# Low parts of all weights on VectorE, a split first weight block, and own slot sequences at both ends of a fused convolution and two-layer kernel

## The chip, the cores and the metric

One core of one Trainium2 chip runs the whole program. The time is that of one execution on the device, in microseconds (us); less is better. Three runs of the kernel before gave 2374.93, 2377.0 and 2377.89 us, so a median of 2377.0 us.

## What is computed

The reference, cut to what matters (`x` is 4 x 4096 x 192, so 16384 tokens of 192 values; the hidden size F is 2048; all float32):

```python
w = softmax(weight)                 # 8 heads, 7 taps
x = causal 7-tap convolution of x along the sequence, one set of taps per group of 24 channels
h = x @ w_in;  x = (h * cos(h)) @ w_out          # layer one, 192 -> 2048 -> 192
h = max(x @ w2_in, 0);  out = (h * h) @ w2_out   # layer two, 192 -> 2048 -> 192
```

## The kernel before

The tokens are cut into 32 tiles of 512 (`TOK`). Channels stand on the partitions; since 192 = 128 + 64, each operand has a main part of 128 rows and a side part of 64.

**Split products.** Every float32 product is made of products of a high and a low part. The high part is a copy of the value in the matmul's type (ScalarE, `ACT.Copy`), the low part is the value minus its high part (a subtraction). Weights are split once: `up_hi`, `up_lo`, `up_side` for the up projection, `dn_hi`, `dn_lo`, `dn_side` for the down projection, with suffix A for layer one and B for layer two. The low parts are made by VectorE for most of layer one (`layer1_up_lo`, `layer1_down_lo`) and by GpSimd for the side of layer one's up weights and for all of layer two (`late_lo_part`). Activations are split for every tile: `g_hi` on ScalarE (L615), `g_lo` on VectorE (L717), and likewise the layer inputs `xin_hi`, `xin_lo`, `xin_side`, `xin_odd`.

**Slots.** The program runs in turns. Turn i works on layer one of tile i (A), layer two of tile i-1 (B), reads and transposes the rows of tile i+1 (X), and transposes back the result of tile i-2 (Y). Turn -1 is the preparation of tile 0, turns 32 and 33 finish layer two and the output. A turn is a list of 18 slots: A 0 to 7 and B 0 to 7, each for two of the 16 blocks of the hidden dimension, and one X and one Y. `SLOTS` gives the order, and `FIRST_SLOTS` that of turns -1 and 0. A slot that doesn't run is passed over. On every engine the instructions stand in program order, slot by slot; semaphores tie the engines together. Turns 3 to 30 are a hardware loop, the others are written out.

**What an engine does in a slot.** TensorE makes the up products of the slot's pair into one of two PSUM buffers `h` (18 matmuls, each of 64 rows by 512 columns) and, interleaved with them on the other half of the rows, the down products (20 matmuls) of the pair that stood four slots earlier (`LAG`). Where only one of the two is there, it runs alone (`up_alone`, `down_alone`) and the two halves of the array overlap in part; `two_up_and_down` joins two ups with one down, and waits for what the second up needs between its steps. ScalarE reads `h` (L594 for A; L596 and the square L598 for B), makes the cosine (L604) one slot later and the high part (L615) two slots later. VectorE makes the fraction of a turn (L703, L705), then the product with the cosine (L712) in the next slot and the low part (L717) in the one after. So three engines pass each A pair round: ScalarE L594, VectorE L703 and L705, ScalarE L604, VectorE L712, ScalarE L615, VectorE L717, TensorE.

**The convolution.** Seven taps on the main and seven on the side part (`tap`, L736 to L744) stand in the slots of `TAP_SLOTS` (`FIRST_TAP_SLOTS` in turns -1 and 0). At `SPLIT_SLOT`, 16, ScalarE copies `x_side_A`, `x_odd` and `x_hi_A` (L651 to L653) and `split_layer1` on VectorE makes `x_lo_A` and the low rows of `x_side_A` (L750, L752); that sets `x1_made`, on which the first up product of the next turn waits. In the same way `split_layer2`, at slot 0, turns layer one's result `y_A` into layer two's input (L759 to L768) and sets `x2_made`, on which B 0 waits.

**The ends.** In turn -1 `layer1_hi` and `late_hi(0)` make the high parts of layer one's weights on ScalarE, as one block each. Layer two's weights come through one staging buffer, `late`: half of the up weights, the other half, the down weights. `late_hi` (ScalarE, at `LATE_SLOTS` of turn 0) and `late_lo_part` (GpSimd) empty it, then SP's queue loads the next part (L293 to L300). In turn 32 only B and Y run, in the places that `SLOTS` gives them.

## Time and profile before

| | |
|---|---|
| median of 3 runs | 2377.0 us |
| profiled execution, its own time | 2377.48 us |
| its span, first to last instruction | 2375.7 us |
| TensorE busy | 2315.7 us (97%), 20352 matmuls |
| VectorE busy | 1902.8 us (80%), 2125 instructions |
| ScalarE busy | 1776.5 us (75%), 1872 instructions |
| GpSimd busy | 24.0 us (1%), 11 instructions |
| mean granted TensorE clock | 0.990 of 2.4 GHz |

The profiled execution is 0.5 us above the median. Busy time of TensorE counts a matmul that runs alone on half of the rows as much as two side by side, so busy is not the same as full. The first two of 40 slices (59.4 us each) show TensorE 0.5 and 0.7 busy, all later ones 0.9 or more but the last (0.8). DMA is 31% busy in the first slice, 10% in the second, and next to nothing after.

### The profile page before, as it was taken

To read this page: it belongs to the slowest core of one execution; us is meant where nothing else is said; L and a number is where in the kernel's file an instruction comes from. 1 tells how busy PE (TensorE), PEld (TensorE's weight loads), DVE (VectorE), ACT (ScalarE), POOL (GpSimd) and SP (SyncE) were. 2 spreads that over 40 slices of the span, in tenths; PEclk is the share of its full clock that TensorE was granted. 3 is DMA by queue.
4 is the path that set the end of the run, shared out by engine and by line. 5 is a ranking of instruction groups with operands and counts; after the bars stand their busy time and mean duration, and the time that the engine had idled before them with its cause. 6 is when DMAs were issued, how large, how long until landed. Compare 5 with 4: busy or idle time off the path is not lost.

```text
span 2375.7 us, 49089 instructions
## 1 busy us (share of the span) xinstructions
PE 2315.7 (97%) x20352; PEld 2163.2 (91%) x20352; DVE 1902.8 (80%) x2125; ACT 1776.5 (75%) x1872; POOL 24.0 (1%) x11
## 2 busy tenths in 40 slices
PE   5699999999999999999999999999999999999998
PEld 4489999999999999999999999999999999999886
DVE  7788788888778878778888878888878888878861
ACT  5377777777777777777777777777777777777764
POOL 1200000000000000000000000000000000000000
PEclk9799999999999999999999999999999999999999
DMA  3100000000000000000000000000000000000000
GB/s 109 37 8 8 14 14 7 13 13 7 13 13 7 13 13 7 13 13 7 13 13 7 13 13 7 13 13 7 13 13 13 7 13 7 13 13 7 7 8 14
DMA packets 39308, 33.05 MB, mean 14 GB/s; under 512 B 1516, under 2 KB 38508, under 8 KB 39020
## 3 DMA queue, kind: packets, MB, share of 16 engines
q1 hardware_dynamic: 39100, 32.58, 4.6%
q8 instruction: 25, 0.41, 0.1%
q14 instruction: 7, 0.06, 0.0%
q10 hardware_dynamic: 176, 0.00, 0.0%
HBM read 19.99 MB, written 12.58 MB: 14 GB/s over the span
## 4 chain that ended last, share of the span: by engine, by line
PE 95%; DVE 3%; ACT 1%; issue 0%; DMA 0%; SPq 0%; ACTq 0%; DVEq 0%
PE h L349 10%; PE h L353 9%; PE h L351 9%; PE h L355 9%; PE y_A L394 6%; PE y_B L388 5%; PE y_B L394 5%; PE y_A L396 5%; PE y_B L396 5%; PE y_B L392 5%; PE y_A L388 5%; PE y_B L390 5%; PE y_A L392 4%; PE y_A L390 4%; PE h L357 3%; PE h L359 2%
## 5 line engine op out<-in xcount | busy, mean ns | idle before, releaser
L717 DVE TENSOR_TENSOR g_lo<-g,g_hi 128x1024 fp32r<-128x1024 f32 x512 | 626.7, 1224 | 200.3 <-ACT g_hi L615 196.4
L615 ACT ACTIVATE g_hi<-g 128x1024 fp32r<-128x1024 f32 x512 | 538.2, 1051 | 49.8 <-DVE g L712 49.5
L604 ACT ACTIVATE w<-w,quarter 128x1024 f32<-128x1024 f32 x256 | 295.5, 1154 | 281.6 <-DVE w L705 281.6
L349 PE MATMUL h<-x_side_A,up_side_A 64*128 64x512 f32 x1024 | 401.6, 395 | 38.2 <-DVE x_side_A L752 29.4
L388 PE MATMUL y_A<-g_hi,dn_lo_A 64*128 64x512 f32 x1024 | 407.5, 398 | 5.1 <-DVE g_lo L717 4.9
L388 PE MATMUL y_B<-g_hi,dn_lo_B 64*128 64x512 f32 x1024 | 405.4, 396 | 2.9 <-DVE g_lo L717 2.4
L394 PE MATMUL y_A<-g_hi,dn_side_A 64*128 64x512 f32 x1024 | 404.8, 395 | 0.0
L349 PE MATMUL h<-x_side_B,up_side_B 64*128 64x512 f32 x1024 | 399.2, 394 | 3.7 <-issue 3.6
L390 PE MATMUL y_A<-g_hi,dn_hi_A 64*128 64x512 f32 x1024 | 402.5, 393 | 0.0
L396 PE MATMUL y_B<-g_lo,dn_side_B 64*128 64x512 f32 x1024 | 400.2, 391 | 0.0
L390 PE MATMUL y_B<-g_hi,dn_hi_B 64*128 64x512 f32 x1024 | 400.2, 391 | 0.0
L396 PE MATMUL y_A<-g_lo,dn_side_A 64*128 64x512 f32 x1024 | 398.9, 390 | 0.0
L394 PE MATMUL y_B<-g_hi,dn_side_B 64*128 64x512 f32 x1024 | 398.4, 389 | 0.2
L392 PE MATMUL y_A<-g_lo,dn_hi_A 64*128 64x512 f32 x1024 | 398.3, 389 | 0.0
L351 PE MATMUL h<-x_hi_A,up_lo_A 64*128 64x512 f32 x1024 | 397.5, 390 | 0.0
L353 PE MATMUL h<-x_lo_A,up_hi_A 64*128 64x512 f32 x1024 | 397.4, 390 | 0.0
L392 PE MATMUL y_B<-g_lo,dn_hi_B 64*128 64x512 f32 x1024 | 397.2, 388 | 0.0
L355 PE MATMUL h<-x_hi_A,up_hi_A 64*128 64x512 f32 x1024 | 397.0, 389 | 0.0
L353 PE MATMUL h<-x_lo_B,up_hi_B 64*128 64x512 f32 x1024 | 393.5, 388 | 0.0
L351 PE MATMUL h<-x_hi_B,up_lo_B 64*128 64x512 f32 x1024 | 393.4, 388 | 0.0
L355 PE MATMUL h<-x_hi_B,up_hi_B 64*128 64x512 f32 x1024 | 393.3, 388 | 0.0
L594 ACT ACTIVATE g<-h 128x1024 f32<-128x1024 f32 x256 | 261.0, 1019 | 128.8 <-PE h L355 127.9
(96 smaller groups left out, 6261.0 us busy)
## 6 DMA issues: line engine op xcount, KB each, us to landing
rows_in<-x SPq DMA_DIRECT2D x32, 384.0 KB, 3.2
...
taps<-weight ACTq DMA_DIRECT2D x4, 0.7 KB
```

Of the source, the lines that this page charges most:

```text
L349: mm = pe.matmul(dst, up_side[kind][rows, f], xin_side[kind][rows, :], start=rows is top, stop=z)
L351: mm = pe.matmul(dst, up_lo[kind][rows, f], xin_hi[kind][rows, :], start=False, stop=z)
L353: mm = pe.matmul(dst, up_hi[kind][rows, f], xin_lo[kind][rows, :], start=False, stop=z)
L355: mm = pe.matmul(dst, up_hi[kind][rows, f], xin_hi[kind][rows, :], start=False, stop=z)
L388: mm = pe.matmul(y[kind][:, 0, :], dn_lo[kind][rows, c, :], hi, start=a, stop=False)
L390: mm = pe.matmul(y[kind][:, 0, :], dn_hi[kind][rows, c, :], hi, start=False, stop=False)
L392: mm = pe.matmul(y[kind][:, 0, :], dn_hi[kind][rows, c, :], lo, start=False, stop=z)
L394: mm = pe.matmul(y[kind][:, 1, :], dn_side[kind][rows, c, :], hi, start=a, stop=False)
L396: mm = pe.matmul(y[kind][:, 1, :], dn_side[kind][rows, c, :], lo, start=False, stop=z)
L604: act.activation(v, v, ACT.Sin, bias=quarter[:, 0:1], scale=-TURN).then_inc(cosine, 1)
L615: act.activation(g_hi[:, r, :, :], g[:, r, :, :], ACT.Copy).then_inc(hi_made[kind], 1)
L717: dve.tensor_tensor(g_lo[:, r, :, :], g[:, r, :, :], g_hi[:, r, :, :].bitcast(F32), ALU.subtract).then_inc(lo_made[kind], 1)
```

## The change

Low parts: the GpSimd block is gone. `late_lo_part` and the subtraction for the side rows of layer one's up weights now stand on VectorE. `late_lo_part(1)`, `(2)` and `(3)` come at slots 8, 11 and 17 of turn 0 (`LATE_LOW_SLOTS`), and `late_hi` moves on ScalarE from slots 9, 12, 15 to 7, 10, 14.

Split block: layer one's up weights are prepared in two parts, the first 512 columns (pairs 0 and 1) and the other 1536. In turn -1 all main taps come before all side taps, ScalarE copies the first part, then `x_hi_A` after the main taps, then the sides, and only then the second part and `late_hi(0)`. TensorE waits for the first part at A 0 and for the second at A 2. The weights are staged in `w` and a new buffer `stage_in_side` instead of `g`.

Input split, in every turn: ScalarE now makes `x_hi_A` first and the two side copies after it, with two increments of `x1_hi`; VectorE makes `x_lo_A` after the first and `x_side_A` after the second.

Slot sequences: `FIRST_SLOTS` and `FIRST_TAP_SLOTS` are changed (turn 0 has its A pairs one slot earlier, X between A 2 and A 3, one tap per slot from 9 to 15), and `LAST_SLOTS` is new, for turns 32 and 33.

```diff
-FIRST_SLOTS = [("B", 0), ("B", 1), ("B", 2), ("B", 3), ("B", 4), ("Y", 0), ("A", 0), ("A", 1), ("A", 2),
-               ("A", 3), ("X", 0), ("A", 4), ("A", 5), ("A", 6), ("A", 7), ("B", 5), ("B", 6), ("B", 7)]
+FIRST_SLOTS = [("B", 0), ("B", 1), ("B", 2), ("B", 3), ("Y", 0), ("A", 0), ("A", 1), ("A", 2), ("X", 0),
+               ("A", 3), ("A", 4), ("A", 5), ("A", 6), ("A", 7), ("B", 4), ("B", 5), ("B", 6), ("B", 7)]
+
+LAST_SLOTS = [("A", 0), ("B", 0), ("B", 1), ("B", 2), ("B", 3), ("B", 4), ("B", 5), ("B", 6), ("B", 7),
+              ("Y", 0), ("A", 1), ("A", 2), ("A", 3), ("A", 4), ("A", 5), ("A", 6), ("A", 7), ("X", 0)]
...
-FIRST_TAP_SLOTS = (11, 11, 12, 13, 14, 15, 15)
+FIRST_TAP_SLOTS = (9, 10, 11, 12, 13, 14, 15)
 SPLIT_SLOT = 16
-LATE_SLOTS = (9, 12, 15)
+LATE_SLOTS = (7, 10, 14)
+LATE_LOW_SLOTS = (8, 11, 17)
+FIRST_PART = 2 * PAIR * P
...
-                if turn.peeled and turn.i == 0 and p == 0:
-                    pe.wait_ge(wi_lo, 2)
+                if turn.peeled and turn.i == 0 and p in (0, 2):
+                    pe.wait_ge(wi_lo, 2 + p)
...
                     if turn.runs("X") and s == SPLIT_SLOT:
 
-                        act.wait_ge(tap_done, (turn.i + 2) * (2 * K))
+                        act.wait_ge(tap_done, (turn.i + 1) * 2 * K + (K if turn.peeled and turn.i == -1 else 2 * K))
                         if turn.runs("A"):
                             act.wait_ge(filled["A"], turn.count("A", NP - 1))
-                        act.activation(xin_side["A"][P - SIDE:P, :], conv_side[P - SIDE:P, :], ACT.Copy)
-                        act.activation(xin_odd[0:SIDE, :], conv_side[P - SIDE:P, :], ACT.Copy)
                         act.activation(xin_hi["A"][:, :], conv[:, :], ACT.Copy).then_inc(x1_hi, 1)
+                        if turn.peeled and turn.i == -1:
+                            act.wait_ge(tap_done, 2 * K)
+                        act.activation(xin_side["A"][low, :], conv_side[low, :], ACT.Copy)
+                        act.activation(xin_odd[top, :], conv_side[low, :], ACT.Copy).then_inc(x1_hi, 1)
+                    if turn.peeled and turn.i == -1 and s == SPLIT_SLOT:
+                        layer1_hi(1)
+                        late_hi(0)
...
-            def layer1_up_lo():
-
-                dve.wait_ge(wi_hi, 2)
-                dve.tensor_tensor(up_lo["A"][:, :], stage_in[:, 0:F], up_hi["A"][:, :].bitcast(F32),
+            def layer1_up_lo(part):
+
+                dve.wait_ge(wi_hi, 2 * part + 2)
+                a, b = (0, FIRST_PART) if part == 0 else (FIRST_PART, F)
+                dve.tensor_tensor(up_lo["A"][:, a:b], stage_in[:, a:b], up_hi["A"][:, a:b].bitcast(F32),
                                   ALU.subtract).then_inc(wi_lo, 1)
+                split = up_side["A"][hi_rows["A"], a:b]
+                dve.tensor_tensor(split, stage_in_side[hi_rows["A"], a:b], split.bitcast(F32),
+                                  ALU.subtract).then_inc(wi_lo, 1)
...
                     if turn.runs("X") and s == SPLIT_SLOT:
-                        if not turn.runs("A"):
-                            layer1_up_lo()
+                        if turn.peeled and turn.i == -1:
+                            layer1_up_lo(0)
                         split_layer1(turn)
-                        if not turn.runs("A"):
+                        if turn.peeled and turn.i == -1:
+                            layer1_up_lo(1)
                             layer1_down_lo()
+                    if turn.peeled and turn.i == 0 and s in LATE_LOW_SLOTS:
+                        late_lo_part(1 + LATE_LOW_SLOTS.index(s))
```

How the instructions stand, at the three places that the prediction speaks of. First VectorE at the end of turn -1, between the taps and the first fraction of tile 0. Before:

```order
L742 SCALAR_TENSOR_TENSOR conv<-xt,taps,conv 128x512 [waits tap_done]
L744 SCALAR_TENSOR_TENSOR conv_side<-xt_side,taps,conv_side 64x512
L686 TENSOR_TENSOR up_lo_A<-g,up_hi_A 128x2048 [waits wi_hi]
L750 TENSOR_TENSOR x_lo_A<-conv,x_hi_A 128x512 [waits x1_hi]
L752 TENSOR_TENSOR x_side_A<-conv_side,x_side_A 64x512
L692 SCALAR_TENSOR_TENSOR dn_lo_A<-late,dn_hi_A 128x2048 [waits late_hi_made]
L695 SCALAR_TENSOR_TENSOR dn_side_A<-late,dn_side_A 128x16x64
```

With the change:

```order
L778 TENSOR_SCALAR conv_side<-xt_side,taps 64x512
L782 SCALAR_TENSOR_TENSOR conv_side<-xt_side,taps,conv_side 64x512 [waits tap_done] x6
L700 TENSOR_TENSOR up_lo_A<-w,up_hi_A 128x512 [waits wi_hi]
L703 TENSOR_TENSOR up_side_A<-stage_in_side,up_side_A 64x512
L788 TENSOR_TENSOR x_lo_A<-conv,x_hi_A 128x512 [waits x1_hi]
L791 TENSOR_TENSOR x_side_A<-conv_side,x_side_A 64x512 [waits x1_hi]
L700 TENSOR_TENSOR up_lo_A<-w,up_hi_A 128x1536 [waits wi_hi]
L703 TENSOR_TENSOR up_side_A<-stage_in_side,up_side_A 64x1536
L723 SCALAR_TENSOR_TENSOR dn_lo_A<-late,dn_hi_A 128x2048 [waits late_hi_made]
L726 SCALAR_TENSOR_TENSOR dn_side_A<-late,dn_side_A 128x16x64
```

The weights of pairs 0 and 1 (512 columns, main and side) are made ahead of the input's low parts, and the other 1536 columns behind them, side rows included.

Then ScalarE at the input split inside the loop. Before:

```order
L586 ACTIVATE late<-h 128x768 [waits rows_stored]
L648 REGISTER_ALU
L651 ACTIVATE x_side_A<-conv_side 64x512 [waits filled_A,tap_done]
L652 ACTIVATE x_odd<-conv_side 64x512
L653 ACTIVATE x_hi_A<-conv 128x512
L615 ACTIVATE g_hi<-g 128x1024 [waits relu_sq,down_top_1_A,down_low_0_A]
```

With the change:

```order
L595 ACTIVATE late<-h 128x768 [waits rows_stored]
L656 REGISTER_ALU
L659 ACTIVATE x_hi_A<-conv 128x512 [waits filled_A,tap_done]
L662 ACTIVATE x_side_A<-conv_side 64x512
L663 ACTIVATE x_odd<-conv_side 64x512
L624 ACTIVATE g_hi<-g 128x1024 [waits relu_sq,down_top_1_A,down_low_0_A]
```

The copy of the main part, `x_hi_A`, has moved ahead of the two side copies.

Last TensorE at the start of turn 32, where layer two's last tile begins. Before, the end of the down products of B 6 of turn 31 and the first up products of B 0:

```order
L388 MATMUL y_B<-g_hi,dn_lo_B 128x512
L390 MATMUL y_B<-g_hi,dn_hi_B 128x512
L392 MATMUL y_B<-g_lo,dn_hi_B 128x512
L349 MATMUL h<-x_side_B,up_side_B 128x512 [waits x2_made,taken_Y]
L351 MATMUL h<-x_hi_B,up_lo_B 128x512
L353 MATMUL h<-x_lo_B,up_hi_B 128x512
L355 MATMUL h<-x_hi_B,up_hi_B 128x512
L357 MATMUL h<-x_side_B,up_even 128x512
```

With the change, the end of the down products of B 5 and what follows:

```order
L396 MATMUL y_B<-g_hi,dn_lo_B 128x512
L398 MATMUL y_B<-g_hi,dn_hi_B 128x512
L400 MATMUL y_B<-g_lo,dn_hi_B 128x512
L357 MATMUL h<-x_side_B,up_side_B 128x512 [waits lo_made_B,x2_made,taken_B]
L396 MATMUL y_B<-g_hi,dn_lo_B 128x512 [waits down_top_0_B]
L359 MATMUL h<-x_hi_B,up_lo_B 128x512
L398 MATMUL y_B<-g_hi,dn_hi_B 128x512
L361 MATMUL h<-x_lo_B,up_hi_B 128x512
L400 MATMUL y_B<-g_lo,dn_hi_B 128x512
```

B 0 used to come alone after both waiting down blocks; now it, and with it its wait for `x2_made`, stands ahead of B 6's down products, which run beside it.

## Rows read from the trace of the kernel before

**Rows 1.** The page, busy time and share of each engine over the span.

```profile
PE 2315.7 (97%) x20352; PEld 2163.2 (91%) x20352; DVE 1902.8 (80%) x2125; ACT 1776.5 (75%) x1872; POOL 24.0 (1%) x11
```

**Rows 2.** Windows: stretch and length, busy time (instructions) by engine, clock, DMA.

```profile
200.00:2250.00 2050.00, 2050.00 (x18367) 1938.63 (x18367) 1694.91 (x1908) 1585.46 (x1674) 0.00 (x0) 1.00 0.04 11
111.20:121.40 10.20, 8.76 (x31) 7.17 (x32) 8.66 (x10) 5.62 (x6) 0.00 (x0) 0.50 0.00 0
2307.40:2368.70 61.30, 58.09 (x379) 46.13 (x375) 14.43 (x15) 30.64 (x32) 0.00 (x0) 0.97 0.02 7
2341.00:2348.00 7.00, 5.27 (x30) 4.27 (x31) 2.36 (x2) 1.40 (x2) 0.00 (x0) 0.76 0.00 0
```

**Rows 3.** Timeline of turn -1: start, duration, engine, line, operation, and idle time before.

```profile
15.75 1.91 ACT L549 ACTIVATE up_side_A<-g 128x2048 fp32r<-128x2048 f32 x1 [7.83 <-DMA g<-w_in]
...
17.72 5.08 DVE L742 SCALAR_TENSOR_TENSOR conv<-xt,taps,conv 128x512 f32<-128x512 f32 x1
17.74 4.51 POOL L823 TENSOR_TENSOR up_side_A<-g,up_side_A 64x2048 fp32r<-64x2048 f32 x1 [17.29 <-ACT up_side_A L549]
...
23.61 2.29 DVE L686 TENSOR_TENSOR up_lo_A<-g,up_hi_A 128x2048 fp32r<-128x2048 f32 x1
...
27.31 0.76 PE L349 MATMUL h<-x_side_A,up_side_A 64*128 64x512 f32 x1 [20.63 <-DVE x_side_A L752]
```

**Rows 4.** Groups of VectorE by line and form, 14 to 102 us.

```profile
L744 DVE SCALAR_TENSOR_TENSOR conv_side<-xt_side,taps,conv_side 64x512 f32<-64x512 f32 x10 | 13.9, 1394 | 0.3
L742 DVE SCALAR_TENSOR_TENSOR conv<-xt,taps,conv 128x512 f32<-128x512 f32 x9 | 13.0, 1447 | 0.2
L712 DVE TENSOR_TENSOR g<-w,g 128x1024 f32<-128x1024 f32 x8 | 12.0, 1498 | 2.8 <-ACT w L604 2.4
L717 DVE TENSOR_TENSOR g_lo<-g,g_hi 128x1024 fp32r<-128x1024 f32 x8 | 10.7, 1339 | 2.3 <-ACT g_hi L615 2.3
L703 DVE TENSOR_SCALAR w<-g 128x1024 f32<-128x1024 f32 x8 | 7.6, 952 | 3.8 <-ACT g L594 3.7
```

**Rows 5.** Timeline of VectorE, fractions of A 0 and A 1 of tile 0.

```profile
34.36 0.69 DVE L703 TENSOR_SCALAR w<-g 128x1024 f32<-128x1024 f32 x1 [3.69 <-ACT g L594]
...
38.67 0.69 DVE L703 TENSOR_SCALAR w<-g 128x1024 f32<-128x1024 f32 x1
```

**Rows 6.** Timeline around the start of turn 1, TensorE and VectorE.

```profile
100.56 0.76 PE L349 MATMUL h<-x_side_A,up_side_A 64*128 64x512 f32 x1 [8.72 <-DVE x_side_A L752]
...
109.68 0.68 DVE L759 TENSOR_TENSOR y_side<-y_A,y_side 64x512 f32<-64x512 f32 x1 [9.22 <-ACT y_side L631]
...
111.86 0.68 DVE L768 TENSOR_TENSOR x_side_B<-y_side,x_side_B 64x512 fp32r<-64x512 f32 x1
```

**Rows 7.** Timeline of the input split in one turn of the loop (turn 15 to 16).

```profile
1240.74 0.63 ACT L653 ACTIVATE x_hi_A<-conv 128x512 fp32r<-128x512 f32 x1
...
1242.11 0.69 DVE L752 TENSOR_TENSOR x_side_A<-conv_side,x_side_A 64x512 fp32r<-64x512 f32 x1
...
1242.67 0.39 PE L359 MATMUL h<-x_odd,up_side_B 64*128 64x512 f32 x1
1242.93 0.49 PE L349 MATMUL h<-x_side_A,up_side_A 64*128 64x512 f32 x1
```

**Rows 8.** Timeline of turns 32 and 33.

```profile
2307.83 1.03 ACT L596 ACTIVATE g<-h 128x1024 f32<-128x1024 f32 x1 [2.67 <-PE h L359]
...
2312.77 0.68 DVE L768 TENSOR_TENSOR x_side_B<-y_side,x_side_B 64x512 fp32r<-64x512 f32 x1
...
2342.77 0.50 PE L388 MATMUL y_B<-g_hi,dn_lo_B 64*128 64x512 f32 x1 [1.73 <-DVE g_lo L717]
...
2361.93 0.46 PE L388 MATMUL y_B<-g_hi,dn_lo_B 64*128 64x512 f32 x1
...
2365.41 0.47 PE L388 MATMUL y_B<-g_hi,dn_lo_B 64*128 64x512 f32 x1
...
2368.78 0.59 ACT L639 ACTIVATE late<-y_B 64x512 f32<-64x512 f32 x1 [6.52 <-PE y_B L392]
```

More of the change, by code:

```diff
@@ L94, in slots @@
     def slots(self, back=0):
-        return FIRST_SLOTS if self.peeled and self.i - back <= 0 else SLOTS
+        if self.peeled and self.i - back <= 0:
+            return FIRST_SLOTS
+        return LAST_SLOTS if self.peeled and self.i - back >= self.tiles else SLOTS
     def pairs(self, back=0):
@@ L185, in tile_program @@
         y_side = sb("y_side", [P, TOK])
+        stage_in_side = sb("stage_in_side", [P, F])
         late = sb("late", [P, NC * D])
@@ L238, in tile_program @@
         hi_made = {k: sem(f"hi_made_{k}") for k in "AB"}
-        stage_in = g[:, :, :, :].rearrange("p r n t -> p (r n t)")
+        stage_in = w[:, :, :, :].rearrange("p r n t -> p (r n t)")
         stage_out = late[:, :].rearrange("p (c d) -> p c d", d=D)
@@ L282, in _ @@
             for half in (0, SIDE):
-                sp.dma_start(stage_in[half:half + SIDE, F:2 * F], w1i[P:D, :]).then_inc(wi_loaded, 16)
+                sp.dma_start(stage_in_side[half:half + SIDE, :], w1i[P:D, :]).then_inc(wi_loaded, 16)
             sp.dma_start(stage_out, w1o.rearrange("(c p) d -> p c d", p=P)).then_inc(late_loaded, 16)
@@ L681, in _, with late_lo_part @@
                               ALU.mult).then_inc(taps_step, 1)
-            def layer1_up_lo():
-                dve.wait_ge(wi_hi, 2)
-                dve.tensor_tensor(up_lo["A"][:, :], stage_in[:, 0:F], up_hi["A"][:, :].bitcast(F32),
+            def layer1_up_lo(part):
+                dve.wait_ge(wi_hi, 2 * part + 2)
+                a, b = (0, FIRST_PART) if part == 0 else (FIRST_PART, F)
+                dve.tensor_tensor(up_lo["A"][:, a:b], stage_in[:, a:b], up_hi["A"][:, a:b].bitcast(F32),
                                   ALU.subtract).then_inc(wi_lo, 1)
+                split = up_side["A"][hi_rows["A"], a:b]
+                dve.tensor_tensor(split, stage_in_side[hi_rows["A"], a:b], split.bitcast(F32),
+                                  ALU.subtract).then_inc(wi_lo, 1)
+            def late_lo_part(n):
+                if n in (1, 2):
+                    cols = slice((n - 1) * HALF, n * HALF)
+                    parts = ((up_lo["B"][:, cols], stage_main, up_hi["B"][:, cols]),
+                             (up_side["B"][hi_rows["B"], cols], stage_side[hi_rows["B"], :],
+                              up_side["B"][hi_rows["B"], cols]))
+                else:
+                    parts = ((dn_lo["B"][:, :, :], stage_out[:, :, 0:P], dn_hi["B"][:, :, :]),
+                             (dn_side["B"][:, :, SIDE:], stage_out[:, :, P:D], dn_side["B"][:, :, 0:SIDE]))
+                for m, (lo, staged, hi) in enumerate(parts):
+                    dve.wait_ge(late_hi_made, 2 * n + 1 + m)
+                    dve.tensor_tensor(lo, staged, hi.bitcast(F32), ALU.subtract).then_inc(late_lo, 1)
             def layer1_down_lo():
@@ L701, in fraction @@
                 v, u = w[:, p % WB, :, :], g[:, r, :, :]
+                if turn.peeled and turn.i == 0 and p == 0:
+                    dve.wait_ge(wi_lo, 4)
                 dve.wait_ge(taken["A"], turn.count("A", p))
@@ L729, in edges, with tap_main @@
                 dve.tensor_copy(tails_side[side, at(t + B), :], xt_side[side, TOK:]).then_inc(edge, 1)
-            def tap(turn, k):
+            def tap_main(turn, k, done):
                 if k == 0:
@@ L789, in body @@
                         edges(turn)
+                    if turn.peeled and turn.i == -1 and s == SPLIT_SLOT:
+                        for k in range(K):
+                            tap_main(turn, k, k)
+                        for k in range(K):
+                            tap_side(turn, k, K + k)
                     for k in range(K):
-                        if turn.runs("X") and s == taps_at[k]:
-                            tap(turn, k)
+                        if turn.runs("X") and s == taps_at[k] and not (turn.peeled and turn.i == -1):
+                            tap_main(turn, k, (turn.i + 1) * (2 * K) + 2 * k)
+                            tap_side(turn, k, (turn.i + 1) * (2 * K) + 2 * k)
                     if kind == "A" and turn.runs("A"):
```

52 lines of the change are left out of this document (18 added, 34 removed).

## The prediction

> **What bounds the kernel now.** I read the shares of the engines first: TensorE is busy 97% of the span, VectorE 80% [rows 1]. Windows then show that this is an average of three stretches. In the loop, between 200 and 2250 us, TensorE is busy every microsecond at the full clock, 2.4 GHz [rows 2], so nothing that only lightens another engine pays there. In the first 113 us it mostly waits, and in the last 61 us (turns 32 and 33) it waits little but runs many blocks alone, on half of the rows. The change works at both ends, and moves one thing in the loop.
>
> In turn -1 TensorE stands 20.6 us until `x_side_A` is there [rows 3]. Ahead of it is VectorE's row of taps, and one tap takes 5.08 us instead of 0.75. It starts within 0.02 us of GpSimd's subtraction and ends 0.5 us after it [rows 3]. The groups of VectorE [rows 4] give the whole of this: with 0.75 us for a tap, 1.23 for L712, 1.22 for L717 and 0.69 for L703, each the undisturbed time of the same instruction, the excess is 6.4, 6.2, 2.2, 0.9 and 2.1 us, together 17.8. Of this 4.3 lie in turn -1, and 13.5 in turn 0, under the six subtractions for layer two. The SBUF page of the Trainium skill (SBUF — State Buffer, Who interferes with whom) says that a VectorE instruction with two SBUF inputs and a GpSimd one that reads SBUF exclude each other for the whole of the first; the trace agrees, a tap lasting to 0.5 us after GpSimd's end.
>
> In turn 0 the three engines pass the A pairs round in single file: the next fraction starts 4.31 us after the last [rows 5], and everything added to VectorE between lengthens it. So the start is bound by VectorE's chain, and the end of it is `x2_made`: B 0 of turn 1 can't start before 112.6 us [rows 6].
>
> **The change, part by part.** I put the sum against the profiled execution (2377.5 us), which is 0.5 us over the median of the runs.
>
> *Turn -1.* Without GpSimd the taps end 4.3 us sooner, at 17.72 + 0.75 + 0.03 + 0.75 = 19.25 us. All main taps first changes no sum, only lets ScalarE start on `x_hi_A`. VectorE then has two pieces of 512 columns at 0.7 us (as `x_side_A`, 0.69 [rows 7]), where there was one of 2.29 [rows 3], then `x_lo_A` and `x_side_A` at 0.7 each: `x1_made` at 22.1, and TensorE starts at 22.2 instead of 27.3. ScalarE's first part is ready at about 15.75 + 1.6 = 17.4 and its side copies at 19.3 + 2 x 0.63 = 20.6, so neither is late. What moves behind is the rest: ScalarE makes the second part from 20.6 to 24.3 (three quarters of 1.91, 1.05 and 1.91), VectorE its two low parts until 27.8 (twice three quarters of 2.29), then the down weights (3.4) until 31.2. TensorE needs the second part at A 2 only, about 29 us. The first fraction starts at 31.2, not 34.36 [rows 5]: **3.2 us** earlier.
>
> *Turn 0.* Before, 66.1 us lie between the first fraction and `x1_made` (100.46, since TensorE starts 0.1 later [rows 6]). Taken away are the 13.5 us of excess. Added are two times two low parts of 1024 columns (1.15 from start to start, as L717) and, after `x1_made`, the down weights' (3.45). That leaves 13.5 - 4.6 = 8.9 us at most. Walked slot by slot: A 0, A 1, A 2 start their fractions at 31.2, 35.5, 39.8; then `late_hi(1)` delays A 2's cosine by 1.2 and `late_lo_part(1)`, the edges and the first tap put A 3's at 50.7; A 4's comes at 56.6 (4.31 and a tap pair of 1.57), A 5's at 62.9 (0.4 late through `late_hi(2)`, whose DMA lands about then), A 6's at 71.0 (with `late_lo_part(2)`), A 7's at 76.9; A 7's low part at 85.0 (behind `late_hi(3)`), the last tap at 86.6, and `x1_made` at 89.3. That is 58.1 us, **8 us** less.
>
> *To B 0 of turn 1.* A 7's down products now run in turn 0's slot 17, at once after its low part. Before, they waited in the queue of turn 1's slot 0 behind `x1_made`, and `x2_made` waited for them. Now VectorE gets to `split_layer2` at 89.3 + 3.4 = 92.7 and needs 2.9 us (109.68 to 112.54 [rows 6]): `x2_made` at 95.6, 17 us earlier. TensorE must also have finished A 0 and A 1, 15 steps each. A step is 0.23 us at 2.4 GHz and 0.43 at 1.2, so they end between 96.3 and 102.2. After B 0 the old run had 1.2 GHz until 121.4 with TensorE busy for 8.8 us [rows 2], which cost 4.4. The gain of the whole start is therefore between 112.6 - 102.2 = 10.4 (low clock as long as before) and 16.3 + 4.4 = 20.7 (high clock throughout); VectorE's chain, 17 us earlier, holds it to about **17**, which I take.
>
> *Loop.* `x1_made` comes 0.7 us sooner, since the two side copies no longer stand ahead of `x_lo_A`: after the last tap three copies and one subtraction instead of three and two. This would be worth nothing if TensorE weren't waiting, but in all 30 turns from 2 on its first A product starts 0.13 us after `x_side_A` ends [rows 7], 0.26 us after the step before where 0.23 is usual, and takes 0.49 instead of 0.39, as after a standstill. So 0.13 us a turn, 30 turns: **4 us**, between 0 and 6.
>
> *Turns 32 and 33.* Before: 6 ups alone (15 steps), 10 downs alone (13 steps), one joined block (28), Y: 248 steps and some in 61.3 us [rows 2]. After: B 5's down alone, two joined blocks (B 0, B 1 with B 6's; B 2, B 3 with B 7's), four full pairs of 19 steps, Y with a down, three downs alone. At 0.2265 a step and 3.5 us for a down alone (2361.93 to 2365.41 [rows 8]): 3.5 + 6.35 + 6.35 + 17.2 + 2.9 + 10.5 = 46.8. New waits: B 0 stands ahead of B 6's down, so TensorE idles from 2310.9 to `x2_made` at 2313.5 [rows 8], 2.6 us, where it used to run that down. At B 4 it waits 2.3 for ScalarE, whose copies of `y_B` (two of 0.6 [rows 8]) come ahead of its read of B 2 (1.03). After a wait of that kind (1.7 us at 2342.77 [rows 8]) the clock fell to 1.2 GHz for 3.4 us, 0.76 over the window of 7 [rows 2], worth 1.7; I count that once, as before. Sum 53.4 against 61.3: **8 us**, between 5 and 10. The clock page of the Trainium skill (TensorE: Matmul & The Clock Gate, Part 1) says that the clock falls only after a whole window of idleness; by that rule both waits would be free, and the tail's gain an estimated 9.7. This case's row shows a fall after 1.7 us, so I don't follow it.
>
> Sum: 17 + 4 + 8 = 29 us, so 2348.5.
>
> **The rivals.** (a) *VectorE's stretched instructions are not GpSimd's doing*, or the work that came over weighs as much. For it: GpSimd took it for nothing in the queue; against it, every stretched instruction lies on a GpSimd one. Then 17.8 us come back at the start, which leaves little of the 17, and 4 + 8 remain: about 2366. (b) *The loop gives nothing*, because the 0.13 us are a block's own seam: 2352.5. (c) *TensorE paces turn 1 at the low clock*, so the start gives 10.4 only: 2355. (d) *Slower.* In the loop ScalarE's new order delays what follows it. `x1_made` has no slack [rows 7]; if the main copy first made the split late, each turn would lose the excess, and the 25 us of both ends would be used up at 0.8 us a turn, about 1.0 for a loss that shows (30 turns, 2382). Against it: three copies of 0.63 us stand there in either order, and the last subtraction needs only the side ones. (e) *The edges of the tail are worse*: two falls of the clock and none gained back: 2352.
>
> **How the numbers follow.** The forecast 0.58, (b) 0.15, (c) 0.12, (e) 0.06, (a) 0.06, (d) 0.03. The range 2339 to 2359 takes in the forecast with its bounds, (b), (c) and (e). A difference of 0.2% (4.8 us) is about what a measurement of this kernel can tell. Faster by more: all but (d), 0.96; the rest 0.02 and 0.02.
>
> **What would show it.** Right: first product at about 22.2 us; no tap over 0.8 us; the first fraction near 31; `x1_made` of turn 1 near 89 and `x2_made` near 96; in the loop a turn of 70.9 instead of 71.0 us, the first A product no longer 0.13 us behind `x_side_A`; from B 7's read in turn 31 (2307.83 [rows 8]) to the `y_B` copy (2368.78) 53 us instead of 61. Wrong: taps still stretched; TensorE, not VectorE, last at B 0 of turn 1; a wait at A 0 in the loop; more than 5 us idle in turn 32.

## The result, and the profile after

| | before | after |
|---|---|---|
| median | 2376.44 us (4 runs, 2374.93 to 2377.89) | 2344.34 us (4 runs, 2343.56 to 2344.38) |
| profiled execution (span) | 2377.48 (2375.7) | 2344.38 (2342.6) |
| granted clock, mean | 0.990 | 0.993 |

The ratio is 0.9864, with a 95% interval of 0.9847 to 0.9881: 32 us faster. The forecast was 2348.5, the range 2339 to 2359. One run of all those below, one of `e6_y1_copy_first`, took 2564.17 us at a granted clock of 0.849, and it counts in the median of its kernel, not in the range beside it.

The page of the kernel after, against [rows 1]: the gap of TensorE fell, and GpSimd is empty.

```profile
PE 2296.1 (98%) x20352; PEld 2029.7 (87%) x20352; DVE 1892.9 (81%) x2134; ACT 1773.3 (76%) x1875; POOL 0.2 (0%) x4
```

**Start.** VectorE in turn -1 of the kernel after (start, duration, operation, idle time before), against [rows 3]:

```profile
14.69 4.68 DVE L782 SCALAR_TENSOR_TENSOR conv_side<-xt_side,taps,conv_side 64x512 f32<-64x512 f32 x6
19.40 0.69 DVE L700 TENSOR_TENSOR up_lo_A<-w,up_hi_A 128x512 fp32r<-128x512 f32 x1
...
21.55 0.69 DVE L791 TENSOR_TENSOR x_side_A<-conv_side,x_side_A 64x512 fp32r<-64x512 f32 x1
24.57 1.76 DVE L700 TENSOR_TENSOR up_lo_A<-w,up_hi_A 128x1536 fp32r<-128x1536 f32 x1 [2.33 <-ACT up_hi_A L561]
...
31.49 0.69 DVE L736 TENSOR_SCALAR w<-g 128x1024 f32<-128x1024 f32 x1
```

Six side taps take 4.68 us, 0.78 each, where the one tap beside GpSimd's subtraction took 5.08. `x_side_A` is made at 22.24 instead of 27.2, and the first fraction starts at 31.49 instead of 34.36 [rows 5]. VectorE's groups over 14 to 102 us of the kernel after, against [rows 4]: every mean is that of the undisturbed instruction.

```profile
L745 DVE TENSOR_TENSOR g<-w,g 128x1024 f32<-128x1024 f32 x9 | 11.0, 1223 | 4.0 <-ACT w L613 3.6
L750 DVE TENSOR_TENSOR g_lo<-g,g_hi 128x1024 fp32r<-128x1024 f32 x9 | 11.0, 1218 | 2.2 <-ACT g_hi L624 2.2
L782 DVE SCALAR_TENSOR_TENSOR conv_side<-xt_side,taps,conv_side 64x512 f32<-64x512 f32 x12 | 9.0, 751 | 0.4
L736 DVE TENSOR_SCALAR w<-g 128x1024 f32<-128x1024 f32 x10 | 6.9, 691 | 0.2
```

Around the start of turn 1, VectorE and TensorE of the kernel after, against [rows 6]: `x1_made` at 88.53 (before 100.46), the down weights' low parts behind it, then `split_layer2` with no wait, `x2_made` at 94.76 (before 112.54), and B 0's first product at 94.87.

```profile
87.84 0.69 DVE L791 TENSOR_TENSOR x_side_A<-conv_side,x_side_A 64x512 fp32r<-64x512 f32 x1 [0.60 <-ACT x_odd L663]
88.56 2.29 DVE L718 TENSOR_TENSOR dn_lo_B<-late,dn_hi_B 128x2048 fp32r<-128x2048 f32 x1
...
94.08 0.68 DVE L807 TENSOR_TENSOR x_side_B<-y_side,x_side_B 64x512 fp32r<-64x512 f32 x1
```

```profile
89.49 0.39 PE L357 MATMUL h<-x_side_A,up_side_A 64*128 64x512 f32 x1
...
94.87 0.47 PE L357 MATMUL h<-x_side_B,up_side_B 64*128 64x512 f32 x1
...
98.90 0.50 PE L357 MATMUL h<-x_side_A,up_side_A 64*128 64x512 f32 x1 [0.25 <-ACT g L603]
...
103.20 0.49 PE L357 MATMUL h<-x_side_B,up_side_B 64*128 64x512 f32 x1 [0.70 <-ACT g L605]
```

The last two rows are waits of TensorE for ScalarE's reads that the kernel before did not have here.

**Loop.** The input split of turn 15 to 16 in the kernel after, against [rows 7]: the last subtraction ends at 1218.53, and the first A product starts 0.67 us later, side by side with B 7's last product (L367), each 0.39 us long.

```profile
1215.89 0.62 ACT L659 ACTIVATE x_hi_A<-conv 128x512 fp32r<-128x512 f32 x1
...
1217.84 0.69 DVE L791 TENSOR_TENSOR x_side_A<-conv_side,x_side_A 64x512 fp32r<-64x512 f32 x1 [0.60 <-ACT x_odd L663]
...
1219.20 0.39 PE L357 MATMUL h<-x_side_A,up_side_A 64*128 64x512 f32 x1
1219.21 0.39 PE L367 MATMUL h<-x_odd,up_side_B 64*128 64x512 f32 x1
```

**Tail.** Turns 32 and 33 of the kernel after, against [rows 8]: TensorE's two waits, at the places foreseen, and the copy of `y_B`.

```profile
2285.29 0.76 PE L357 MATMUL h<-x_side_B,up_side_B 64*128 64x512 f32 x1 [2.91 <-issue]
...
2303.01 0.49 PE L357 MATMUL h<-x_side_B,up_side_B 64*128 64x512 f32 x1 [2.27 <-ACT g L605]
...
2335.93 0.59 ACT L648 ACTIVATE late<-y_B 64x512 f32<-64x512 f32 x1 [8.89 <-PE y_B L400]
```

Windows of the kernel after, against [rows 2] (stretch and length, busy time of PE, PEld, DVE, ACT, POOL, clock, DMA): the loop is as full as before; the start of turn 1 runs at 2.4 GHz where it had 1.2; the tail has a mean clock of 0.90, where it had 0.97.

```profile
200.00:2250.00 2050.00, 2050.00 (x18436) 1817.21 (x18434) 1696.40 (x1907) 1589.12 (x1682) 0.00 (x0) 1.00 0.04 11
88.50:96.00 7.50, 7.50 (x51) 6.42 (x51) 7.34 (x10) 2.22 (x3) 0.00 (x0) 0.97 0.01 2
2279.50:2340.50 61.00, 52.00 (x389) 41.99 (x385) 15.20 (x16) 32.20 (x35) 0.00 (x0) 0.90 0.02 7
2282.60:2290.60 8.00, 5.31 (x26) 4.53 (x28) 3.75 (x6) 1.26 (x2) 0.00 (x0) 0.57 0.01 2
2298.60:2306.60 8.00, 5.74 (x42) 4.33 (x40) 2.09 (x3) 5.69 (x7) 0.00 (x0) 0.85 0.00 0
```

**Where the time went.** Two TensorE events cut both traces at the same places of the program: the first A product of turn 2 (177.98 before, 158.78 after) and of turn 31 (2236.97, 2208.81). The third is the first copy of `y_B` (2368.78, 2335.93).

| | before | after | gain | forecast |
|---|---|---|---|---|
| to turn 2 | 177.98 | 158.78 | 19.2 | 17 (10.4 to 20.7) |
| turn 2 to turn 31, 29 turns | 2058.99 | 2050.03 | 9.0 | 4 (0 to 6) |
| turn 31 to the `y_B` copy | 131.81 | 127.12 | 4.7 | 8 (5 to 10) |

With 0.2 us behind the copy this is the 33.1 us between the two spans.

### The profile page after: what moved, and what is told of

It is laid out like the page before. It is cut to its first block, busy times and chain, and to the rows that moved or that the text cites. A ratio compares the mean times of both kernels' runs of the same rounds, so it can differ in the third digit from the quotient of the medians.

```text
span 2342.6 us, 49150 instructions
## 1 busy us (share of the span) xinstructions
PE 2296.1 (98%) x20352; PEld 2029.7 (87%) x20352; DVE 1892.9 (81%) x2134; ACT 1773.3 (76%) x1875; POOL 0.2 (0%) x4
## 4 chain that ended last, share of the span: by engine, by line
PE 95%; DVE 3%; ACT 1%; issue 1%; DMA 0%; SPq 0%; DVEq 0%; ACTq 0%
PE h L357 10%; PE h L359 10%; PE h L361 10%; PE h L363 10%; PE y_A L402 6%; PE y_A L404 5%; PE y_B L402 5%; PE y_B L404 5%; PE y_A L396 5%; PE y_B L396 5%; PE y_B L400 5%; PE y_A L400 4%; PE y_A L398 4%; PE y_B L398 4%; PE h L367 2%; PE h L365 2%
## 5 line engine op out<-in xcount | busy, mean ns | idle before, releaser
L624 ACT ACTIVATE g_hi<-g 128x1024 fp32r<-128x1024 f32 x512 | 538.7, 1052 | 57.4 <-DVE g L745 56.6
L357 PE MATMUL h<-x_side_A,up_side_A 64*128 64x512 f32 x1024 | 396.2, 390 | 21.7 <-DVE x_side_A L791 15.5
L359 PE MATMUL h<-x_hi_A,up_lo_A 64*128 64x512 f32 x1024 | 395.4, 388 | 0.0
L359 PE MATMUL h<-x_hi_B,up_lo_B 64*128 64x512 f32 x1024 | 393.3, 388 | 0.0
## 6 DMA issues: line engine op xcount, KB each, us to landing
late<-w_out SPq DMA_DIRECT2D x2, 1536.0 KB, 10.4
```

The lines of the kernel that those rows point to most:

```text
L357: mm = pe.matmul(dst, up_side[kind][rows, f], xin_side[kind][rows, :], start=rows is top, stop=z)
L359: mm = pe.matmul(dst, up_lo[kind][rows, f], xin_hi[kind][rows, :], start=False, stop=z)
L624: act.activation(g_hi[:, r, :, :], g[:, r, :, :], ACT.Copy).then_inc(hi_made[kind], 1)
```

## The experiments

All times are medians beside runs of the kernel before on the same chip (2377.1 to 2377.6 us). The questions were three: is the gain of the loop the order of ScalarE's copies and nothing else, and why 0.31 us a turn? What of the start is GpSimd, and what the new slots? And what did the tail lose?

### The loop: the order of the copies

`e1_old_copy_order` is the kernel after with the old order of copies in turns 0 to 30.

```diff
-                        act.activation(xin_hi["A"][:, :], conv[:, :], ACT.Copy).then_inc(x1_hi, 1)
                         if turn.peeled and turn.i == -1:
...
+                        else:
+                            act.activation(xin_side["A"][low, :], conv_side[low, :], ACT.Copy)
+                            act.activation(xin_odd[top, :], conv_side[low, :], ACT.Copy).then_inc(x1_hi, 1)
+                            act.activation(xin_hi["A"][:, :], conv[:, :], ACT.Copy).then_inc(x1_hi, 1)
...
-                dve.wait_ge(x1_hi, turn.i * 2 + 3)
+                dve.wait_ge(x1_hi, turn.i * 2 + (3 if turn.peeled and turn.i == -1 else 4))
```

So VectorE again waits for all three copies before its first subtraction.

> The changed kernel (2344.3 us) with one thing undone: in turns 0 to 30 ScalarE copies the two side parts first and x_hi_A last, as before. Theory: the shorter turn of the loop (70.69 us against 71.00 before) comes from x1_made being 0.7 us earlier, so this run goes back to a turn of 71.0, the first A product stands 0.13 us behind x_side_A again, and the time is 2344.3 + 28 x 0.31 = 2353. Rival: the shorter turn comes from something else (buffers at other addresses, GpSimd gone), then the turn stays 70.69 and the time 2344 to 2345.

Measured: 2354.59 us (2353.72 to 2355.0), ratio 0.9905, 95% [0.9889, 0.9922], so 10.3 us over the kernel after. A turn takes 71.02 us again (mean of turns 3 to 30, from first A product to first A product). VectorE and TensorE at the split of this kernel:

```profile
1223.17 0.69 DVE L792 TENSOR_TENSOR x_lo_A<-conv,x_hi_A 128x512 fp32r<-128x512 f32 x1 [1.43 <-ACT x_hi_A L667]
1223.88 0.69 DVE L795 TENSOR_TENSOR x_side_A<-conv_side,x_side_A 64x512 fp32r<-64x512 f32 x1
```

```profile
1224.39 0.39 PE L367 MATMUL h<-x_odd,up_side_B 64*128 64x512 f32 x1
1224.69 0.49 PE L357 MATMUL h<-x_side_A,up_side_A 64*128 64x512 f32 x1
```

VectorE waits 1.43 us for the main copy and then does both subtractions; the first A product starts 0.12 us behind the second, and 0.30 behind L367, beside which it stood.

`e2_before_new_copy_order` is the kernel before with only the new order.

```diff
-                        act.activation(xin_side["A"][P - SIDE:P, :], conv_side[P - SIDE:P, :], ACT.Copy)
-                        act.activation(xin_odd[0:SIDE, :], conv_side[P - SIDE:P, :], ACT.Copy)
                         act.activation(xin_hi["A"][:, :], conv[:, :], ACT.Copy).then_inc(x1_hi, 1)
+                        act.activation(xin_side["A"][P - SIDE:P, :], conv_side[P - SIDE:P, :], ACT.Copy)
+                        act.activation(xin_odd[0:SIDE, :], conv_side[P - SIDE:P, :], ACT.Copy).then_inc(x1_hi, 1)
...
-                dve.wait_ge(x1_hi, turn.i + 2)
+                dve.wait_ge(x1_hi, turn.i * 2 + 3)
...
+                dve.wait_ge(x1_hi, turn.i * 2 + 4)
```

> The kernel before (2376.4 us) with that one edit alone: x_hi_A first, two increments of x1_hi. Theory: turn 70.69 instead of 71.00, 8.7 us over 28 turns, and 0.7 more at each of the two starts: about 2367. Rival: no change in the loop, 2375 to 2376.

Measured: 2366.52 us (2365.12 to 2366.96), ratio 0.9957 [0.9941, 0.9974], 10.6 us under the kernel before, with a turn of 70.66. On its TensorE the two products start together, as in the kernel after:

```profile
1235.72 0.39 PE L349 MATMUL h<-x_side_A,up_side_A 64*128 64x512 f32 x1
1235.73 0.39 PE L359 MATMUL h<-x_odd,up_side_B 64*128 64x512 f32 x1
```

So the order of three copies is worth 10.3 to 10.6 us in either kernel. Of this about 9.7 us lie in the loop (0.33 us a turn). Kernels whose loops are the same differ by 0.02 us a turn (70.66 to 70.69), so smaller differences say nothing. What a late `x_side_A` costs, the next three kernels measure: the kernel after with redundant work ahead of the last subtraction, in turns 3 to 30, written to a buffer that nobody reads. The edit (512 columns; the others have 256, or twice 512):

```diff
                 dve.wait_ge(x1_hi, turn.i * 2 + 4)
+                if not turn.peeled:
+                    dve.tensor_tensor(stage_in_side[:, 0:512], conv[:, 0:512], conv[:, 0:512],
+                                      ALU.subtract)
                 dve.tensor_tensor(xin_side["A"][0:SIDE, :], conv_side[side, :],
```

> The changed kernel with one more subtraction of 256 columns (about 0.42 us) ahead of x_side_A's on VectorE, in turns 3 to 30, into a buffer that nothing reads. x_side_A is ready 0.67 us before the first A product in the changed kernel, 0.13 of which is the signal's way, so 0.54 us are free. Theory: the turn stays 70.69 us, time 2344. Rival (every delay of x1_made lengthens the turn): 71.1 us, 2356.

> As before, 512 columns (0.72 us). Theory: 0.18 us over what is free, and a standstill's restart of about 0.15 on top (the turn of the kernel before, 0.70 us later, is 0.31 longer): turn 71.0 us, 28 turns, 2353. Rival without a restart: 70.87 us, 2349.

> As before, two subtractions of 512 columns (1.44 us). Theory: 0.90 us over and the same restart: turn 71.7 us, 2373. If the restart grows with the wait, more; if the wait costs only itself, 71.6 us, 2370.

| `x_side_A` later by | turn | more than the kernel after's 70.69 | delay less 0.54 | time |
|---|---|---|---|---|
| 0.43 us | 70.68 | none | none | 2343.12 (2 runs) |
| 0.71 us | 70.86 | 0.17 | 0.17 | 2347.11 (2 runs) |
| 1.31 us | 71.48 | 0.79 | 0.77 | 2365.33 (2364.34 to 2366.01) |

The 0.54 us are read from the kernel after: `x_side_A` ends 0.67 ahead of the product, and in the kernel before, where the product waits, 0.13 pass between the two (1242.80 to 1242.93). The split of the kernel with 0.71 us more, VectorE and then TensorE:

```profile
1220.14 0.69 DVE L792 TENSOR_TENSOR stage_in_side<-conv 128x512 f32<-128x512 f32 x1 [0.60 <-ACT x_odd L663]
1220.85 0.69 DVE L794 TENSOR_TENSOR x_side_A<-conv_side,x_side_A 64x512 fp32r<-64x512 f32 x1
```

```profile
1221.51 0.39 PE L367 MATMUL h<-x_odd,up_side_B 64*128 64x512 f32 x1
1221.67 0.49 PE L357 MATMUL h<-x_side_A,up_side_A 64*128 64x512 f32 x1
```

A wait costs its length past the slack, and hardly anything for standing still. The product behind it does have a record of 0.49 instead of 0.39 us, but of the 0.1 at most 0.02 show in the turn. The 70.86 of the second kernel is the reading without a restart's price (70.87). The 71.48 of the third lie under both expectations (71.7 and 71.6), since its delay is 1.31 us and not 1.44; they are what the slack of 0.54 gives. The times of the second and third are 2 and 1 us less than 28 turns at this price would make; their ends ran 2.4 us shorter (the table of the tail below).

### The start: GpSimd and the slots

`e8_before_low_on_vector` is the kernel before with one change: GpSimd's seven subtractions run on VectorE, the one for layer one at the end of `layer1_up_lo`, the six for layer two in slots 10, 13 and 17.

```diff
+                    if turn.peeled and turn.i == 0 and s in (10, 13, 17):
+                        late_lo_part(1 + (10, 13, 17).index(s))
...
-        @block.gpsimd
-        def _(pool):
```

> The kernel before (2377) with the GpSimd block's seven subtractions moved to VectorE and nothing else (slots, copies, order of the taps as before; layer two's at slots 10, 13 and 17 of turn 0). Theory: turn -1 loses the stretch of 4.3 us and gains one subtraction of 2.2, turn 0 loses 13.5 us of stretches and gains 4.6 ahead of x1_made; x2_made of turn 1 comes 2.1 + 8.9 = 11 us earlier, at 101.5, time 2366. Rival (the work weighs as much as the stretches): x2_made at 108 or later, time 2372 to 2377.

Measured: 2365.51 us (2364.16 to 2366.36), ratio 0.9955 [0.9939, 0.9972], 11.6 us under the kernel before. `x1_made` of turn 1 comes at 89.61, `x2_made` at 101.44 (101.5 was expected). VectorE there:

```profile
88.92 0.69 DVE L769 TENSOR_TENSOR x_side_A<-conv_side,x_side_A 64x512 fp32r<-64x512 f32 x1
...
91.85 1.22 DVE L704 TENSOR_TENSOR dn_side_B<-late,dn_side_B 128x1024 fp32r<-128x1024 f32 x1
98.58 0.68 DVE L776 TENSOR_TENSOR y_side<-y_A,y_side 64x512 f32<-64x512 f32 x1 [5.52 <-ACT y_side L631]
```

No tap of this kernel is over 0.76 us. Rival (a) is refuted: the stretching is GpSimd's doing, and the work that came over weighs less. GpSimd was busy 24.0 us with it [rows 1]. VectorE needs 1.22 to 2.29 us for each of the seven, 10.7 us in all (five of 1.22 for 1024 columns is 6.1, two of 2048 columns 4.6), and 17.8 come back. `x2_made` came as expected, 11.1 us earlier, but the two parts did not. In turn -1 the first fraction is only 0.4 us earlier (33.97) and not 2.1, since VectorE there stands 1.99 us for ScalarE's `up_hi_A`. Turn 0 is 10.5 us shorter (66.1 before, 55.6 now) and not 8.9: VectorE had 1.13 us idle at 57.03 in the kernel before, and the added work fills that. The row of 98.58 also shows what is left: VectorE stands 5.52 us until A 7's down products, behind `x1_made` in TensorE's queue, have given `y_A`. That is what the new slot sequence takes away.

`e3_late_low_on_gpsimd` is the kernel after with the six subtractions for layer two back on GpSimd.

```diff
-                    if turn.peeled and turn.i == 0 and s in LATE_LOW_SLOTS:
-                        late_lo_part(1 + LATE_LOW_SLOTS.index(s))
...
+        @block.gpsimd
+        def _(pool):
...
+            for n in range(1, 1 + len(LATE_SLOTS)):
+                late_lo_part(n)
```

> The changed kernel with the six low parts of layer two's weights on GpSimd again (the side of layer one's stays on VectorE). Theory (GpSimd and VectorE shut each other out): VectorE instructions that start beside a GpSimd subtraction are stretched by 13 us in all, against 8.1 us that leave VectorE's queue, so x2_made of turn 1 comes 1 to 6 us later and the time is 2345 to 2350. Rival (no exclusion): no VectorE instruction is stretched, x2_made comes up to 8 us earlier, and the time is 2337 to 2340.

Measured: 2351.46 us (2351.06 to 2352.6), ratio 0.9893 [0.9876, 0.9909], 7.1 over the kernel after and outside the expectation; `x2_made` at 103.33, 8.6 later where 1 to 6 were expected. Two of GpSimd's rows, and the VectorE instructions that start on them:

```profile
85.46 4.54 POOL L850 TENSOR_TENSOR dn_lo_B<-late,dn_hi_B 128x2048 fp32r<-128x2048 f32 x1 [22.50 <-ACT dn_hi_B L576]
89.96 2.79 POOL L850 TENSOR_TENSOR dn_side_B<-late,dn_side_B 128x1024 fp32r<-128x1024 f32 x1
```

```profile
85.53 5.02 DVE L768 SCALAR_TENSOR_TENSOR conv_side<-xt_side,taps,conv_side 64x512 f32<-64x512 f32 x1
90.58 3.25 DVE L736 TENSOR_TENSOR g_lo<-g,g_hi 128x1024 fp32r<-128x1024 f32 x1
```

A tap that starts 0.07 us after GpSimd takes 5.02 instead of 0.75, and the next instruction 3.25 instead of 1.22. In all the stretched groups exceed their undisturbed times by 13.7 us (12 x 0.54 for L768, 8 x 0.37 for L736, 8 x 0.28 for L731, 8 x 0.26 for L722), nearly the 13.5 of turn 0 in the kernel before. Of VectorE's own 8.1 us for this work only 4.6 stand ahead of `x1_made`, so the balance there is 13.7 - 4.6 = 9.1 us: 9.4 were measured (97.96 against 88.53). The 6 us that I gave as the most are about what is left when all 8.1 are set against it.

`e5_old_first_slots` gives the kernel after the slot sequence that the first tile had before, with the tap and late slots that go with it.

```diff
-FIRST_SLOTS = [("B", 0), ("B", 1), ("B", 2), ("B", 3), ("Y", 0), ("A", 0), ("A", 1), ("A", 2), ("X", 0),
-               ("A", 3), ("A", 4), ("A", 5), ("A", 6), ("A", 7), ("B", 4), ("B", 5), ("B", 6), ("B", 7)]
+FIRST_SLOTS = [("B", 0), ("B", 1), ("B", 2), ("B", 3), ("B", 4), ("Y", 0), ("A", 0), ("A", 1), ("A", 2),
+               ("A", 3), ("X", 0), ("A", 4), ("A", 5), ("A", 6), ("A", 7), ("B", 5), ("B", 6), ("B", 7)]
```

> The changed kernel with the old slot sequence and tap slots for turns -1 and 0 (late_hi at 9, 12, 15 again, the subtractions on VectorE at 10, 13, 17). Forecast from the rows: the walk through turn 0 loses what the new order gave beside GpSimd's absence. A 7's down products wait behind x1_made again, so x2_made follows x1_made by 12 us (as before) instead of 6, and B 0 of turn 1 comes 6 us or more later: 2350 to 2355. Rival: the order is worth nothing beside the missing stretches, 2344 to 2346.

Measured: 2348.10 us (2346.45 to 2348.68), ratio 0.9875 [0.9858, 0.9891], 3.8 over the kernel after, 2 us under the expectation. `x1_made` comes even 2.1 us earlier (86.41), but `x2_made` only 13.2 us behind it, at 99.61. The reason is in VectorE's row:

```profile
96.74 0.68 DVE L798 TENSOR_TENSOR y_side<-y_A,y_side 64x512 f32<-64x512 f32 x1 [6.87 <-ACT y_side L640]
```

So the new sequence makes `x1_made` 2.1 us later and `x2_made` 4.9 earlier. VectorE's wait of 6.87 us for A 7's down products, which the kernel after does not have, is what it takes away; what the places of X, of the taps and of the late parts do in it was not taken apart. The first A product of turn 2 comes at 164.09, 5.3 us later than in the kernel after. The time shows 3.8, because this trace's loop (0.7 us) and end (0.7 us, less time at 1.2 GHz) are shorter.

### The tail: the order of the last blocks

`e4_old_last_slots` is the kernel after without its own sequence for the last layer-two turn.

```diff
-        return LAST_SLOTS if self.peeled and self.i - back >= self.tiles else SLOTS
+        return SLOTS
```

> The changed kernel without the slot sequence for turns 32 and 33 (they use the loop's). Theory: the tail from B 7's read in turn 31 to the copy of y_B takes 61 us again instead of 56.4, time 2349. Of the 8 us forecast, 3.4 were lost to the clock (6.8 and 3.4 us at 1.2 GHz against 3.4 us before). Rival: the tail's gain is not the sequence's, time 2344.

Measured: 2348.19 us (2347.21 to 2348.34), ratio 0.9878 [0.9862, 0.9895], 3.9 over the kernel after (2349 was expected). Here the new sequence is worth 4 us, not 8.

How much it is worth depends on the clock, and the other runs show it. Seven kernels of this study have the same instructions in turns 32 and 33 and the same two waits (2.91 to 2.93 us at B 0, 2.24 to 2.27 at B 4). The profiled executions differ in the stretches at 1.2 GHz behind these waits:

| kernel | at 1.2 GHz behind B 0's wait | behind B 4's | turn 31 to the `y_B` copy |
|---|---|---|---|
| after | 6.8 us | 3.4 | 127.1 |
| `e1_old_copy_order` | 6.8 | 3.4 | 127.5 |
| `e3_late_low_on_gpsimd` | 3.4 | 3.4 | 126.2 |
| `e5_old_first_slots` | 3.4 | 3.4 | 126.4 |
| `d1_delay_256` | 3.4 | 3.4 | 126.3 |
| `d2_delay_512` | 3.4 | none | 124.7 |
| `d3_delay_1024` | 3.4 | none | 124.8 |

With the old sequence this stretch takes 131.8 us in each of the four kernels that have it, so the new one gives 4.3 to 7.1 us. Windows of `d2_delay_512` around its waits, which end at 2290.16 and 2307.03:

```profile
2289.00:2297.00 8.00, 6.84 (x46) 6.25 (x48) 2.27 (x3) 0.58 (x1) 0.00 (x0) 0.79 0.01 2
2305.70:2313.70 8.00, 6.67 (x58) 5.56 (x60) 2.91 (x3) 7.91 (x9) 0.00 (x0) 1.00 0.01 2
```

`e6_y1_copy_first` moves, in turn 32 alone, ScalarE's two copies of `y_A` (0.59 and 0.60 us) ahead of its work for B 7, to the end of turn 31; so `x2_made` comes sooner and B 0 waits less.

```diff
-                    if s == 0 and turn.runs("A", 1):
+                    if turn.peeled and turn.i == turn.tiles - 1 and s == NS - 1:
...
+                        act.activation(y_side[0:SIDE, :], y["A"][SIDE:P, 1, :], ACT.Copy).then_inc(y1_copied, 1)
+                        act.activation(xin_hi["B"][:, :], y["A"][:, 0, :], ACT.Copy).then_inc(y1_copied, 1)
+                    if s == 0 and turn.runs("A", 1) and not (turn.peeled and turn.i == turn.tiles):
```

> The changed kernel with one move in turn 31: ScalarE copies layer one's result y_A before it reads and squares B 7, not after. Theory of the tail: TensorE's 2.9 us wait at B 0 of turn 32 is this chain, 2.1 us of it are the read and the square, and the 6.8 us at 1.2 GHz that follow it come from the wait. The wait shrinks to under 1 us, and with it the stretch at half clock goes: 2.1 + 3.4 = 5.5 us, 2339. If the clock falls in any case: 2342. Rival (the wait hides something else that is late, such as B 6's low part): 2344.

Measured: 2339.99 us, ratio 0.9843 [0.9823, 0.9862] (2339.38 to 2340.14). This is 4.4 us under the kernel after, and the fastest version of this study. The waits of TensorE in its tail, and the windows at both places:

```profile
PE h L357 <- ACT g L605: 2.2, 1, 2.2
...
PE h L357 <- issue: 0.9, 1, 0.9
```

```profile
2277.60:2285.60 8.00, 7.13 (x58) 5.90 (x56) 4.03 (x6) 4.23 (x5) 0.00 (x0) 1.00 0.00 0
2293.60:2301.60 8.00, 5.76 (x38) 4.42 (x36) 1.91 (x2) 5.95 (x7) 0.00 (x0) 0.80 0.00 0
```

The wait at B 0 went from 2.9 to 0.9 us, and the clock did not fall there. In the kernel after, TensorE was busy at 1.2 GHz from 2285.3 to 2290.6, 5.3 us, which is 2.7 us lost. Wait and clock together are 4.7, of which 4.4 arrived. The 2.0 us of the wait are seen nearly by themselves: `d2_delay_512`, which like this kernel has one stretch of 3.4 us at 1.2 GHz in its tail, takes 124.7 us from turn 31 to the `y_B` copy, and this kernel 122.7. That the missing stretch at B 0 comes from the shorter wait is likely and not proven: behind the wait of 2.9 us the clock fell in all seven kernels of the table, behind that of 0.9 us in neither of the two that have it.

`e7_y1_first_y2_late` also lets ScalarE's copies of `y_B` stand one slot later, so that its read of B 2 isn't behind them.

```diff
-                    if s == 3 and turn.runs("Y"):
+                    if s == (4 if turn.peeled and turn.i == turn.tiles else 3) and turn.runs("Y"):
```

> As the run before, and in turn 32 ScalarE copies y_B one slot later, after it has read B 2. Theory: the wait of 2.3 us at B 4 falls to 1.3, since B 2's buffer is free at once and only the copies and VectorE's sum remain; with a shorter wait the second stretch at half clock (3.4 us, 1.7 lost) may go too: 1.0 to 2.7 us less than the run before, 2336.5 to 2338. Rival: the later copies hold up B 3's read and square and so B 5, no gain.

Measured: 2340.79 us (2340.5 to 2341.34), ratio 0.9847 [0.983, 0.9863]: nothing gained, as the rival said. ScalarE around the copies, and the wait that took the old one's place:

```profile
2294.21 1.02 ACT L605 ACTIVATE g<-h 128x1024 f32<-128x1024 f32 x1 [1.21 <-PE h L367]
...
2296.23 1.04 ACT L624 ACTIVATE g_hi<-g 128x1024 fp32r<-128x1024 f32 x1
2297.30 0.59 ACT L654 ACTIVATE late<-y_B 64x512 f32<-64x512 f32 x1
```

```profile
PE h L357 <- DVE late L830: 2.7, 1, 2.7
```

One slot later also means behind the read, the square and the high part that lie in that slot, 3.1 us in all. The copies start at 2297.30, and B 4, which needs `y_B`'s space, waits 2.7 us for them instead of 2.2 for the read.

## Why the prediction was right, and where not

**Turn -1: right.** The first fraction came at 31.49 (31.2), the first product at 22.29 (22.2). No wait showed up that the sum didn't have.

**Turn 0: right, within a us at each step, by a walk that was 1 us too long.** The fractions of A 3 to A 7 were forecast at 50.7, 56.6, 62.9, 71.0 and 76.9 and came at 50.74, 56.61, 62.49, 70.45 and 76.32; `x1_made` at 88.53 (89.3), `x2_made` at 94.76 (95.6). The chain of VectorE with undisturbed durations explains the stretch. From the first fraction to `x1_made` it took 57.0 us, 9.1 less than the 66.1 before. The walk had said 8 and the plain balance "8.9 us at most", and even that was a little low: part of the added work ran in time in which VectorE had stood idle.

**To B 0 of turn 1: 19.2 instead of 17.** The failed step is "VectorE's chain, 17 us earlier, holds it to about 17". The chain came 17.8 us earlier (`x2_made`), and it does not hold the gain: what the clock gives back comes on top, and that sum put it at nothing. TensorE ran at 2.4 GHz from about 89.0 on (0.97 over 88.5 to 96), and both pairs ran from 89.49 with B 0 joining at 94.87 while the last steps of A 1 still went. The kernel before lost 4.4 us to the clock behind its B 0, and this one nothing. So the gain comes near the upper bound, 20.7. Of the 1.5 us short of it, 1.0 are the two waits for ScalarE's reads at 98.90 and 103.20. Rival (c), which put 10.4 here, didn't occur.

**The loop: 9.0 instead of 4, and outside its bounds.** The mechanism was right, as both kernels with the copies exchanged show. The mis-sized term is "0.26 us after the step before where 0.23 is usual", with "So 0.13 us a turn" drawn from it. I took the wait against the product before it in time, which is a neighbour in the other half of the rows. An A product would have started beside B 7's last one (1242.67 [rows 7]), as 1219.20 stands beside 1219.21 in the kernel after; it started at 1242.93, 0.26 us later; over the 29 turns that wait it is 0.28 on average (0.25 to 0.29), where the kernel after has its A product 0.01 ahead. That is 0.29 of the 0.31 us that the turn loses, and 29 turns of 0.31 are the 9.0 us. Turn 2 of the kernel before did not wait (its product at 177.98 and L359 at 178.07), so 29 turns count and not 30. The longer record, counted as 0.1 of the 0.13, is not the price, as the delays showed, and rival (b) was wrong too: at a seam without a wait nothing is lost. Also `x1_made` came 0.81 us sooner after B 6's read than before (6.32 against 7.13), where I had 0.70: 0.54 us of it isn't used. Rival (d), the slower side, didn't come about; its mechanism is real, though: `x_side_A` later by 1.31 us costs 0.79 a turn, and 21 us in all.

**The tail: 4.7 instead of 8, just under its bound of 5.** The walk of the blocks and both waits were right (2.6 and 2.3 forecast, 2.91 and 2.27 measured). The failed step is "I count that once, as before". TensorE ran at 1.2 GHz for 6.8 us from 2283.7 (5.3 of them busy) and for 3.4 us from 2304.2, worth 2.7 and 1.7; I had 1.7. With the 0.3 of the longer wait this is 3.0 of the missing 3.3. In `d2_delay_512` and `d3_delay_1024` the clock did fall once only, and there the same tail gives 7.1 and 7.0 us. So the walk was sound to 1 us, and what the clock adds is not the program's alone: by the table above it differs between executions of the same instructions. Rival (e) had part of the truth: two falls, but with them a gain. The clock page of the Trainium skill (TensorE: Matmul & The Clock Gate, Part 1) would have given an estimated 9.7 by its rule, under which waits as short as these leave the clock alone; the measurement went the other way, as the row of the kernel before had said.

The three errors, +2.2, +5.0 and -3.3, leave 4 us of 33. The total was so close partly by luck, because they cancel: two of the three parts lie outside their own bounds. Single parts, each measured by itself, are 11.6 (GpSimd's work moved), 10.3 to 10.6 (copies), 3.8 (first slots) and 3.9 (last slots), together about 30 of 32. The rest, some 2 us, could be the split of the first weights' block, which no kernel tried alone; it is no more than what the clock in the tail alone moves between executions.
